# Exchanging real and imaginary state rows with a VectorE stream shuffle, two units at a time

## The chip, the cores and the metric

The kernel runs on one NeuronCore of a Trainium2 chip. The metric is the device time of one execution in microseconds (us). TensorE is called PE, VectorE DVE, ScalarE ACT, GpSimd POOL, and SP issues most of the DMAs.

## What is computed

Three layers follow one another: a gated linear attention with a complex decaying state, a mixture of experts that sends each token to one of 8 experts, and a bilinear layer. The change touches the first:

```python
# B=2, H=8, S=768, D=48; a is scaled to |a| <= 0.999
for t in range(S):
    new_re = ar * S_re - ai * S_im
    new_im = ar * S_im + ai * S_re
    S_re, S_im = new_re + outer(k[t], v[t]), new_im
    y[t] = q[t] @ S_re
x = moe(y)            # x @ w_gate, argmax, two matmuls per expert
out = (x @ w_a) * (x @ w_b) @ w_out
```

## The kernel before

The sequence is cut into 8 chunks of 96 steps, so there are 128 rows of (batch, head, chunk). A first stage on DVE (with ACT and PE helping) scans the decay factors inside all chunks at once (`scan`, L365) and multiplies keys and queries by them (`product`, L415 to L437). A product writes 12 time steps of 96 channels: for each step first 48 real numbers, then 48 imaginary ones. There are 16 products of 1152 elements per partition, one of them cut in three. The products are turned on PE so that the 96 channels lie on the partitions (`turn`, L454), and those of the keys also go to HBM (`x_rows`) and come back per chunk (`load_x`, L716).

The second stage, which this document calls the state stage, goes through 32 units of four heads; two successive units (n even, n + 1) share a chunk and a batch and are called a pair here, pairs 0 to 15. Pairs 0 to 7 belong to batch 0, pairs 8 to 15 to batch 1; the first pair of a batch (0 and 8) has no incoming state, the last (7 and 15) makes no outgoing one. The loop is at L876 to L928. What a unit does:

- `scores` (L696): 4 matmuls, keys times queries inside the chunk, issued one unit ahead; `masked` (L706): DVE masks them into SBUF.
- `state_in` (L821): 4 matmuls, keys times values; DVE adds the old state (L839, or copies where there is none, L841) into `zm[0]`, 96 partitions x 224.
- The state is multiplied by the chunk's complex decay. The real factor: DVE `zm[1] = zm[0] * Wr` (L910). The imaginary factor needs real and imaginary rows exchanged, with a sign: PE multiplies `zm[0]` by the constant matrix `swap` (`turned_state`, L869 to L874), DVE multiplies the result by `Wi` (L925), and DVE adds both into `Z[gr]` (L928), the state for the next chunk.
- `queried` (L844): 4 matmuls of masked scores with values, and for each, where a state came in, one of queries with the state (L857). ACT copies the outcome to SBUF (L865, L866).

Once a pair is finished, the tokens of its chunk are routed: DVE picks the expert (`choose`, L725), PE counts ranks (`ranks`, L746), DVE makes the slots (`place_chunk`, L756), and a POOL indirect DMA scatters the rows to `sorted_x` (L781). Routing of chunk 13 is followed by a load of expert 0's first rows from `sorted_x` (L919 to L921), which `turn_first` (L785) waits for at the end of the stage. Chunks 14 and 15 are added by `add_late`. Then the experts and the bilinear layer run, mostly on PE.

The order on each engine is the program order written out by hand in the loop; every engine works its queue in order and waits on semaphores. The decay factors of whole chunks, `Wr` and `Wi`, come from `end_factors` (L656), six DVE operations on `eT`, which ACT copied from PSUM (L607).

Of the kernel before, what the change touches and what calls it, by code (L numbers as in the profile page):

```python
# [24 lines left out]
ALU = mybir.AluOpType  # L25
# [43 lines left out]
def build(nc, dims, qk, v, vt, a, w_gate, w1, w2, wa, wb, wo, out, CAP):  # L69
    B, H, S, D = dims  # L70
    P = 128
# [31 lines left out]
    with ctx:  # L103
# [3 lines left out]
        def sb(name, shape, dt=F32, at=ctx, side="left"):  # L107
# [15 lines left out]
        swap = sb("swap", [C2, C2])  # L123
# [15 lines left out]
        m = pool.done(g.memset(swap[:], 0.0))  # L139
        pool.wait(m)  # L140
# [27 lines left out]
        with att:  # L168
# [86 lines left out]
            dve.done(vv.tensor_copy(trib[:], tri[:]))  # L255
            m_const = [dve.done(vv.tensor_scalar(baseb[:], basef[0:L], ident[0:L, 0:1], None, ALU.mult))]
# [158 lines left out]
            def product(s, x, n, cuts=1):  # L415
# [8 lines left out]
                for u in range(cuts):  # L424
# [3 lines left out]
                    m = dve.done(tt(walk(o, [D, 2], [2 * D if n else -2 * D, w], [1, D]),  # L428
# [165 lines left out]
            dve.done(vv.tensor_copy(ends[:, 2:4, :].rearrange("p i (r d) -> p i r d", r=2),  # L594
                                    walk(AT_Z[1] + lo_at + D, [SA, 2], [0, 2], [1, D])))
            dve.wait(m)
            dve.done(tt(ends[:, 0, :].rearrange("p (r d) -> p r d", r=2), both(tmp[:, 0, :]), both(tmp[:, 2, :]), ALU.add))
            m_ends = dve.done(tt(ends[:, 1, :].rearrange("p (r d) -> p r d", r=2), both(tmp[:, 3, :]),
# [8 lines left out]
            m_eT = act.done(ss.activation(eT[0:C2], bank[b][0:C2, :].rearrange("p (i q) -> p i q", i=4), ACT.Copy))  # L607
# [16 lines left out]
            AT_ST = AT_ZM + 3 * YB * DE  # L624
            AT_XS = AT_ST + NU * YB * DE
# [3 lines left out]
            zm = [flat(AT_ZM + i * YB * DE, YB * DE, C2) for i in range(3)]  # L629
            ws = [flat(AT_ENDS + i * P, P, C2) for i in range(2)]  # L630
            Z = [flat(AT_ST + i * YB * DE, YB * DE, C2) for i in range(NU)]
# [45 lines left out]
            z_done = [None] * NU  # L677
            rk = bank[0][:, 0:E]
            m_lgp, m_lx = {}, []

# [755 lines left out]
```

## Time and profile before

| | us |
|---|---|
| median of 3 runs | 593.72 (592.88 to 594.88) |
| profiled execution, time | 594.27 |
| profiled execution, span | 593.0 |
| PE busy | 548.9 (93%) |
| DVE busy | 375.5 (63%) |
| ACT busy | 266.0 (45%) |
| POOL busy | 51.8 (9%) |

The granted PE clock is 0.972 of full speed over the span. Up to about 118 us the first stage runs, from 120.5 to 218 us the state stage, then experts and the bilinear layer. Busy time is an average over stages with different limits, so the state stage has to be read by itself.

### The profile page before, as it was taken

To read this page: it belongs to the slowest core of one execution; us is meant where nothing else is said; L and a number is where in the kernel's file an instruction comes from. 1 tells how busy PE (TensorE), PEld (TensorE's weight loads), DVE (VectorE), ACT (ScalarE), POOL (GpSimd) and SP (SyncE) were. 2 spreads that over 40 slices of the span, in tenths; PEclk is the share of its full clock that TensorE was granted. 3 is DMA by queue.
4 is the path that set the end of the run, shared out by engine and by line. 5 is a ranking of instruction groups with operands and counts; after the bars stand their busy time and mean duration, and the time that the engine had idled before them with its cause. 6 is when DMAs were issued, how large, how long until landed. Compare 5 with 4: busy or idle time off the path is not lost.

```text
span 593.0 us, 10227 instructions
## 1 busy us (share of the span) xinstructions
PE 548.9 (93%) x3800; PEld 488.6 (82%) x3801; DVE 375.5 (63%) x938; ACT 266.0 (45%) x566; POOL 51.8 (9%) x66
## 2 busy tenths in 40 slices
PE   0499697889999999999999999999999999999996
PEld 0267364779999998999999998888888888888886
DVE  5999999968888869888889886534412212122121
ACT  5665665822222237777778784433232122322112
POOL 1000000001121116000000000350020000200002
PEclk9977897999999989999999999999999999999999
DMA  8999032497222125966666629730010000100001
GB/s 312 274 384 338 1 156 67 177 265 216 71 68 65 42 72 159 324 237 207 200 229 214 204 90 162 138 103 0 1 55 0 1 0 1 54 1 0 1 0 54
DMA packets 46321, 73.28 MB, mean 124 GB/s; under 512 B 16520, under 2 KB 38792, under 8 KB 45384
## 3 DMA queue, kind: packets, MB, share of 16 engines
q1 hardware_dynamic: 44360, 67.97, 37.0%
q0 software_dynamic: 1920, 4.75, 2.5%
q8 instruction: 28, 0.46, 0.3%
q14 instruction: 13, 0.11, 0.1%
HBM read 55.76 MB, written 16.97 MB: 123 GB/s over the span
## 4 chain that ended last, share of the span: by engine, by line
PE 79%; DVE 11%; ACT 4%; DMA 3%; issue 2%; POOL 1%; DVEq 0%; POOLq 0%; SPq 0%; ACTq 0%
PE psum L1330 26%; PE psum L1303 12%; PE psum L1136 11%; PE psum L1099 9%; PE psum L855 4%; PE psum L702 3%; PE psum L829 3%; PE psum L283 2%; PE psum L857 2%; PE psum L284 2%; DVE region L375 2%; PE psum L874 2%; DMA xrow<-sorted_x 2%; DVE region L428 2%; DVE region L380 1%
## 5 line engine op out<-in xcount | busy, mean ns | idle before, releaser
L1345 DVE TENSOR_TENSOR ga<-ga,psum 128x512 f32<-128x512 f32 x36 | 24.8, 688 | 129.8 <-PE psum L1330 124.7
L1349 ACT ACTIVATE gh<-ga 128x512 fp32r<-128x512 f32 x36 | 22.8, 632 | 80.7 <-DVE ga L1345 73.9
L1343 ACT ACTIVATE ga<-psum 128x512 f32<-128x512 f32 x36 | 21.5, 598 | 76.0 <-PE psum L1330 74.6
L283 PE MATMUL psum<-region,ident 128*128 128x384 f32 (+1 forms) x42 | 25.2, 692 | 32.7 <-ACT region L293 22.9
L1136 PE MATMUL psum<-hh,w2h 128*128 128x224 f32 x192 | 53.7, 279 | 0.0
L1099 PE MATMUL psum<-xh,w1h 128*128 128x224 f32 x192 | 53.0, 276 | 0.5 <-DVE xl L970 0.5
L1136 PE MATMUL psum<-hh,w2l 128*128 128x224 f32 x192 | 52.7, 274 | 0.0
L1099 PE MATMUL psum<-xh,w1l 128*128 128x224 f32 x192 | 52.7, 274 | 0.0
L1099 PE MATMUL psum<-xl,w1h 128*128 128x224 f32 x192 | 52.7, 274 | 0.0
L1136 PE MATMUL psum<-hl,w2h 128*128 128x224 f32 x192 | 52.6, 274 | 0.0
L1303 PE MATMUL psum<-woh,gh 128*128 128x384 f32 x144 | 48.3, 335 | 0.4 <-DVE gl L1351 0.4
L1303 PE MATMUL psum<-wol,gh 128*128 128x384 f32 x144 | 48.2, 335 | 0.0
L1303 PE MATMUL psum<-woh,gl 128*128 128x384 f32 x144 | 48.1, 334 | 0.0
L283 PEld LDWEIGHTS psum<-region,ident 128*128 128x128 f32 x42 | 10.6, 270 | 41.1 <-issue 21.3
L1330 PE MATMUL psum<-yh,wah 128*128 128x512 f32 x108 | 42.9, 397 | 0.0
L1330 PE MATMUL psum<-yh,wbh 128*128 128x512 f32 x108 | 42.8, 396 | 0.0
L1330 PE MATMUL psum<-yl,wah 128*128 128x512 f32 x108 | 42.8, 396 | 0.0
L1330 PE MATMUL psum<-yh,wal 128*128 128x512 f32 x108 | 42.6, 395 | 0.0
L1330 PE MATMUL psum<-yl,wbh 128*128 128x512 f32 x108 | 42.6, 395 | 0.0
L1330 PE MATMUL psum<-yh,wbl 128*128 128x512 f32 x108 | 42.6, 395 | 0.0
L1351 DVE TENSOR_TENSOR gl<-ga,gh 128x512 fp32r<-128x512 f32 x36 | 24.9, 693 | 25.2 <-ACT gh L1349 24.5
L1099 PEld LDWEIGHTS psum<-xh,w1h 128*128 128x128 f32 x192 | 36.9, 192 | 0.8 <-DVE xl L970 0.7
(198 smaller groups left out, 1461.4 us busy)
## 6 DMA issues: line engine op xcount, KB each, us to landing
raw<-w SPq DMA_DIRECT2D x14, 1536.0 KB, 6.7
sorted_x<-region SPq DMA_DIRECT2D x8, 579.0 KB, 13.7
queries<-qk SPq DMA_DIRECT2D x4, 1152.0 KB, 25.7
xrow<-sorted_x SPq DMA_DIRECT2D x7, 579.0 KB, 6.8
region<-x_rows SPq DMA_DIRECT2D x14, 288.0 KB
queries<-w SPq DMA_DIRECT2D x2, 1536.0 KB, 15.1
x_rows<-region SPq DMA_DIRECT2D x5, 576.0 KB, 2.8
region<-a SPq DMA_DIRECT2D x2, 1152.0 KB, 9.9
```

What stands on the lines that cost most here:

```text
L283: nc.tensor.matmul(x, ident[:], x0[:, cut], start=True, stop=False)
L702: m = nc.tensor.matmul(bank[2 + r][0:L, i * L:(i + 1) * L], XT[:, p, :], QT[:, p, :], start=True, stop=True)
L829: m = nc.tensor.matmul(bank[6][0:C2, i * DE:i * DE + 2 * D], XS[x_at % NXS][:, n % XB * YB + i, :], with_gate(p), start=True, stop=True)
L855: m = nc.tensor.matmul(o, SC[r][:, i, :], with_gate(p), start=True, stop=j == 0)
L1099: m = nc.tensor.matmul(bank[b][:, 0:cols], wx[:, c, f * P:(f + 1) * P], xx[:, c, 0:cols], start=c == 0 and i == 0, stop=c == KC - 1 and i ...
L1136: m = nc.tensor.matmul(bank[YB0 + c][:, 0:cols], wx[:, f, c * P:(c + 1) * P], xx[:, f, 0:cols], start=f == 0 and i == 0, stop=f == NF - 1 ...
L1303: m = nc.tensor.matmul(ot[s][:, 0:DM], gx[f % GB3][:, s * P:(s + 1) * P], wx[:, f, :], start=f == 0 and i == 0, stop=f == NF2 - 1 and i == 2)
L1330: m = nc.tensor.matmul(b_[:, 0:TT], wx[:, f, c, :], xx[:, c, t * TT:(t + 1) * TT], start=c == 0 and i == 0, stop=c == KC - 1 and i == 2)
L1343: m = act.done(ss.activation(ga[f % 2][:], ba[:, 0:TT], ACT.Copy))
L1345: m = dve.done(tt(ga[f % 2][:], ga[f % 2][:], bb[:, 0:TT], ALU.mult))
L1349: m = act.done(ss.activation(gh[f % GB3][:], ga[f % 2][:], ACT.Copy))
L1351: m_g.append(dve.done(tt(gl[f % GB3][:], ga[f % 2][:], z32(gh[f % GB3][:]), ALU.subtract)))
```

## The change

The sixteen products write real and imaginary parts interleaved (channel 2d real, 2d + 1 imaginary), as do the factors in `ends`. Real and imaginary partners are then neighbouring partitions, and DVE's stream shuffle with the lane list `i ^ 1` exchanges them; the matrix `swap`, its building on POOL, and the matmul are gone. The sign is put into the imaginary decay factor: `eT` is copied in two ACT operations, one with the per-partition scale `sign`. Two units are handled at once: the add, the shuffle, the imaginary product and the last add have 448 elements instead of 224, and the real product is done by ACT, in eight operations of 56 elements, each with a per-partition scale. `end_factors` moves in front of the first `masked`, the waits for the values behind the first two `scores`. In the loop, both `state_in` of a pair come first, the state's last add (`state_out`) moves into the second unit, and the ranks and slots of chunk 13 move ahead of `queried`.

```diff
-        swap = sb("swap", [C2, C2])
+        sign = sb("sign", [C2, C2])
...
-        m = pool.done(g.memset(swap[:], 0.0))
-        pool.wait(m)
+        pool.wait(m_ones)
...
-        c = pool.done(g.affine_select(out=swap[:], in_=swap[:], compare_op=ALU.not_equal, fill=1.0, base=-D,
-                                      pattern=[[-1, C2]], channel_multiplier=1))
-        pool.wait(c)
-        c_swap = pool.done(g.affine_select(out=swap[:], in_=swap[:], compare_op=ALU.not_equal, fill=-1.0, base=D,
-                                           pattern=[[-1, C2]], channel_multiplier=1))
...
+            SHUFFLE = [i ^ 1 for i in range(32)]
+            m = dve.done(vv.tensor_reduce(out=sign[:, 1:2], in_=ident[0:C2, 1:C2:2], axis=AXX, op=ALU.add))
+            dve.wait(m)
+            m_sign = dve.done(vv.tensor_scalar(sign[:, 0:1], sign[:, 1:2], -2.0, 1.0, ALU.mult, ALU.add))
...
-                    m = dve.done(tt(walk(o, [D, 2], [2 * D if n else -2 * D, w], [1, D]),
+                    m = dve.done(tt(walk(o, [1, 2], [2 * D if n else -2 * D, w], [2, D]),
                                     walk(AT_Z[1] + s * W + n * D + i0 * PAIR, [SA, 2], [PAIR, w], [1, D]),
                                     walk(k_at + i0 * PAIR, [0, 2], [PAIR, w], [1, D]), ALU.mult))
...
-            m_eT = act.done(ss.activation(eT[0:C2], bank[b][0:C2, :].rearrange("p (i q) -> p i q", i=4), ACT.Copy))
+            act.wait(m_sign)
+            by_i = bank[b][0:C2, :].rearrange("p (i q) -> p i q", i=4)
+            act.done(ss.activation(eT[0:C2, 0:4:2, :], by_i[:, 0:4:2, :], ACT.Copy))
+            m_eT = act.done(ss.activation(eT[0:C2, 1:4:2, :], by_i[:, 1:4:2, :], ACT.Copy, scale=sign[:, 0:1]))
...
-            nc.tensor.wait_ge(s_v[0], 16)
-            nc.tensor.wait_ge(s_vwin[0], 16)
-            pe.wait(c_swap)
+            m_factors = end_factors()
...
+            def added(n):
+
+                dve.wait(m_u[n + 1])
+                if units[n][0]:
+                    dve.wait(z_done[n - GB], m_zr[n - GB])
+                    m_add[n] = dve.done(tt(z_sum, Z[(units[n][0] - 1) % 2], state, ALU.add))
+                else:
+                    if m_zr:
+                        dve.wait(m_zr[max(m_zr)])
+                    m_add[n] = dve.done(vv.tensor_copy(z_sum, state))
+                act.wait(m_add[n], m_factors)
+                if z_done:
+                    act.wait(z_done[max(z_done)])
+                for r in range(GB):
+                    for i, p in enumerate(heads(n + r)):
+                        m_zr[n] = act.done(ss.activation(z_re[:, r, i, :], z_sum[:, r, i, :], ACT.Copy,
+                                                         scale=Wr[:, p:p + 1]))
+
+            def turned(n):
+
+                j, gr = units[n]
+                dve.wait(m_add[n])
+                m = dve.done(vv.stream_shuffle(z_im, z_sum, SHUFFLE))
+                dve.wait(m)
+                w = Wi[:, gr * YB * NC + j:(gr + GB) * YB * NC:NC].rearrange("c (r i) -> c r i", r=GB)
+                m_zi[n] = dve.done(tt(z_im, z_im, w.unsqueeze(3).broadcast_to([C2, GB, YB, DE]), ALU.mult))
+
+            def state_out(n):
+
+                dve.wait(m_zi[n], m_zr[n])
+                z_done[n] = dve.done(tt(Z[units[n][0] % 2], z_re, z_im, ALU.add))
...
-            def turned_state(n):
-
-                pe.wait(m_add[n])
-                if m_turned_z:
-                    pe.wait(m_turned_z)
-                return pe.done(nc.tensor.matmul(bank[7][0:C2, 0:YB * DE], swap[:], zm[0], start=True, stop=True))
...
+                if n == 0:
+                    nc.tensor.wait_ge(s_v[0], 16)
+                    nc.tensor.wait_ge(s_vwin[0], 16)
+                if more and n % GB == 0:
+                    for i in range(GB):
+                        state_in(n + i)
+                    added(n)
+                if n + 1 < NUNIT:
+                    masked(n + 1)
+                if n % GB == 0 and done == LATE - 1:
                     ranks(done)
                     place_chunk(done)
+                    first_rows()
+                if more and n % GB == 0:
+                    turned(n)
+                if n % GB and n > GB and done < LATE - 1:
+                    place_chunk(done)
+                if more and n % GB:
+                    state_out(n - 1)
+                queried(n)
+                if n % GB == 0 and n and done != LATE - 1:
                     ranks(done)
-                if more:
-                    m_j = turned_state(n)
-                    dve.wait(m_j)
-                    m_turned_z = m_jd[n] = dve.done(tt(z3[2], bank[7][0:C2, 0:YB * DE].rearrange("p (i e) -> p i e", i=YB),
-                                                       wv(Wi), ALU.mult))
-                    dve.wait(m_jd[n], m_zr, m_y[n])
-                    z_done[gr] = dve.done(tt(z3[3], z3[1], z3[2], ALU.add))
+                    if done >= LATE:
+                        place_chunk(done)
```

## Rows read from the trace of the kernel before

**Rows 1.** The page's chain that ended last, shares of the span.

```profile
PE 79%; DVE 11%; ACT 4%; DMA 3%; issue 2%; POOL 1%; DVEq 0%; POOLq 0%; SPq 0%; ACTq 0%
```

**Rows 2.** Busy us (xinstructions) by window: pairs 1-6, 8, 9, 10-13; clock, DMA, GB/s.

```profile
127.91:166.07 38.16, 38.16 (x426) 37.54 (x425) 32.34 (x121) 7.76 (x36) 4.79 (x5) 1.00 0.54 158
...
170.29:175.37 5.08, 5.08 (x58) 4.98 (x57) 3.92 (x17) 1.51 (x8) 1.39 (x2) 1.00 0.11 32
175.37:181.96 6.59, 6.58 (x72) 6.34 (x71) 5.82 (x22) 1.36 (x8) 0.93 (x1) 1.00 0.34 87
181.96:207.44 25.48, 25.48 (x286) 25.06 (x284) 21.48 (x81) 5.31 (x25) 3.68 (x4) 1.00 0.20 55
```

**Rows 3.** PE in order of time, inside pair 4: start, duration, operation.

```profile
146.55 0.58 PE L874 MATMUL psum<-region,swap 96*96 96x224 f32 x2
146.97 0.84 PE L702 MATMUL psum<-region 96*96 96x96 f32 x8
...
148.32 0.33 PE L855 MATMUL psum<-region 96*96 96x96 f32 x2
...
149.65 0.58 PE L874 MATMUL psum<-region,swap 96*96 96x224 f32 x2
```

**Rows 4.** DVE in order of time, same pair; brackets: idle before, releaser.

```profile
147.90 0.26 DVE L729 TENSOR_REDUCE route<-region 96x8 f32<-96x64 f32 x1
...
148.97 0.38 DVE L839 TENSOR_TENSOR region<-region,psum 96x224 f32<-96x224 f32 x1
...
151.62 0.38 DVE L839 TENSOR_TENSOR region<-region,psum 96x224 f32<-96x224 f32 x1 [0.55 <-PE psum L829]
151.93 0.15 DVE L760 TENSOR_TENSOR so<-so,ohb 96x8 bf16<-96x8 bf16 x1
...
152.52 0.38 DVE L910 TENSOR_TENSOR region<-region 96x224 f32<-96x224 f32 x1
```

**Rows 5.** DVE in order of time at the state stage's start.

```profile
119.39 0.69 DVE L473 COPY region<-psum 96x512 f32<-96x512 f32 x1 [1.59 <-PE psum L465]
...
124.08 0.57 DVE L712 COPY_PREDICATED region<-mask,psum 96x384 f32<-96x384 int32 x1
124.55 0.27 DVE L658 TENSOR_TENSOR region<-region 96x127 f32<-96x127 f32 x1
```

**Rows 6.** DVE groups by form: xcount, busy us, mean ns of one, idle before.

```profile
L428 DVE TENSOR_TENSOR region<-region,queries 128x1152 f32<-128x1152 f32 x10 | 13.1, 1352 | 0.1
...
L928 DVE TENSOR_TENSOR region<-region 96x224 f32<-96x224 f32 x28 | 10.9, 388 | 1.0
...
L729 DVE TENSOR_REDUCE route<-region 96x8 f32<-96x64 f32 x16 | 4.1, 258 | 1.6 <-ACT region L865 1.6
...
L1272 DVE TENSOR_REDUCE gate<-past 128x12 f32<-128x96 f32 x1 | 0.3, 253 | 0.0
...
L1355 DVE TENSOR_SCALAR gate<-tag 128x12 f32<-128x12 f32 x1 | 0.2, 167 | 0.0
```

**Rows 7.** ACT groups by form, the same columns.

```profile
L1179 ACT ACTIVATE yh<-psum 128x384 f32 x24 | 10.3, 492 | 18.3 <-PE psum L1099 13.7 <-PE psum L1136 4.6
...
L1375 ACT ACTIVATE raw<-psum,gate 128x384 f32<-128x384 f32 x12 | 6.6, 582 | 6.5 <-PE psum L1303 6.5
...
L865 ACT ACTIVATE region<-psum 96x32 f32<-96x32 f32 x32 | 6.2, 193 | 54.7 <-PE psum L857 45.5 <-PE psum L855 9.2
```

**Rows 8.** PE in order of time at the stage's start and at pair 1.

```profile
120.51 1.57 PE L702 MATMUL psum<-region 96*96 96x96 f32 x16 [1.16 <-DMA region<-vw_rows]
...
127.91 0.84 PE L702 MATMUL psum<-region 96*96 96x96 f32 x8
```

**Rows 9.** The chain of waits at the stage's end: start, us, what.

```profile
212.09 2.56 DMA sorted_x<-region,sloti
...
214.72 3.84 DMA region<-sorted_x
```

**Rows 10.** PE in order of time, the first operation after those loads.

```profile
218.60 2.93 PE L791 MATMUL psum<-ident,region 128*128 128x128 f32 x12 [0.62 <-DMA region<-sorted_x]
```

More of the change, by code:

```diff
@@ L628, in build @@
             maski = mask[:].bitcast(I32).unsqueeze(1).broadcast_to([L, YB, L])
-            zm = [flat(AT_ZM + i * YB * DE, YB * DE, C2) for i in range(3)]
+            z_sum, z_re, z_im = (flat(AT_ZM + i * PW, PW, C2).rearrange("p (r i e) -> p r i e", i=YB, e=DE) for i in range(3))
             ws = [flat(AT_ENDS + i * P, P, C2) for i in range(2)]
-            Z = [flat(AT_ST + i * YB * DE, YB * DE, C2) for i in range(NU)]
+            Z = [flat(AT_ST + i * PW, PW, C2).rearrange("p (r i e) -> p r i e", i=YB, e=DE) for i in range(2)]
+            state = psum[0:C2, 6:8, 0:YB * DE].rearrange("p r (i e) -> p r i e", i=YB)
             X = flat(AT_Z[1], TAU * ROW, L).rearrange("p (t c) -> p t c", c=ROW)
@@ L671, in build @@
             assert GB == XB and B == 2
-            m_scored, m_sc, m_u, m_y, m_yx, m_add, m_jd = ({} for _ in range(7))
+            m_scored, m_sc, m_u, m_y, m_yx, m_zr, m_zi, m_add = ({} for _ in range(8))
             m_oh, m_slot, m_rk, m_tk, m_so, m_hot, m_part_x, m_read_lg = ({} for _ in range(8))
@@ L828, in state_in @@
                 for i, p in enumerate(heads(n)):
-                    m = nc.tensor.matmul(bank[6][0:C2, i * DE:i * DE + 2 * D],
-                                         XS[x_at % NXS][:, n % XB * YB + i, :], with_gate(p),
-                                         start=True, stop=True)
+                    m = nc.tensor.matmul(bank[6 + r][0:C2, i * DE:i * DE + 2 * D], XS[x_at % NXS][:, r * YB + i, :],
+                                         with_gate(p), start=True, stop=True)
                 m_u[n] = pe.done(m)
-                if n % XB == XB - 1 and x_at + NXS < NX:
+                if r == GB - 1 and x_at + NXS < NX:
@@ L851, in queried @@
                 if j:
-                    pe.wait(z_done[gr])
+                    pe.wait(z_done[n - r - GB])
                 for i, p in enumerate(heads(n)):
@@ L893, in build @@
                         sp.dma_start(y.rearrange("p (c f) -> p c f", f=x.shape[-1]), x).then_inc(s_, 16)
-                if more and n:
-                    state_in(n)
-                if n % GB == 1 and n > GB and done < LATE - 1:
+                if n == 0:
[5 more added lines that the diff above has]
+                    added(n)
@@ L897, in build @@
+                if n + 1 < NUNIT:
+                    masked(n + 1)
+                if n % GB == 0 and done == LATE - 1:
                     ranks(done)
                     place_chunk(done)
-                if n == 0:
-                    queried(0)
-                    state_in(0)
-                    masked(1)
-                    m_ends = end_factors()
-                z3 = [x.rearrange("p (i e) -> p i e", i=YB) for x in (*zm, Z[gr])]
-                def wv(x):
-                    return x[:, gr * YB * NC + j:(gr + 1) * YB * NC:NC].unsqueeze(2).broadcast_to([C2, YB, DE])
@@ L908, in build @@
-                if more:
-                    dve.wait(m_add[n], m_ends)
-                    m_zr = dve.done(tt(z3[1], z3[0], wv(Wr), ALU.mult))
-                if n:
-                    if n + 1 < NUNIT:
-                        masked(n + 1)
-                    queried(n)
-                if n % GB == 0 and done >= LATE - 1:
-                    ranks(done)
-                    place_chunk(done)
-                    if done == LATE - 1:
-                        sp.wait_ge(pe.sem, m_y[NUNIT // 2 - 1][1])
-                        sp.wait_ge(s_sc, 16 * LATE)
-                        sp.dma_start(rows_0, sorted_x[0, 0:CAP, :].rearrange("(i p) c -> p i c", p=P)).then_inc(s_row0, 16)
@@ L990, in build @@
             pe_done, dve_done = (pe, pe_chunks, False), (dve, dve_chunks, False)
-            act.wait(m_y[NUNIT - 1], *z_done)
-            dve.wait(*z_done)
+            act.wait(m_y[NUNIT - 1], *z_done.values())
+            dve.wait(*z_done.values())
             nc.scalar.wait_ge(s_w1, 16)
```

33 lines of the change are left out of this document (15 added, 18 removed).

## The prediction

> **What bounds the kernel now.** I read the shares of the chain that ended last first, then the state stage by windows, then single engines in order of time inside one pair. PE holds 79% of the chain and DVE 11% [rows 1]. In the state stage PE is busy in all of 38.16 us of pairs 1 to 6 and all of 25.48 us of pairs 10 to 13, at full granted clock, so a pair costs 6.36 to 6.37 us [rows 2]. DVE is busy 32.34 of 38.16 us (85%), and in each pair it idles 0.55 us for a PE result [rows 4]: it is behind PE, but not far. What the exchange costs on PE is the step from one `swap` matmul to the next work, 146.55 to 146.97, 0.42 us, twice in a pair [rows 3]. A group of four 96x96 matmuls costs 0.68 us (two groups in 146.97 to 148.32), a `queried` with incoming state 1.33 us (148.32 to 149.65) [rows 3]. Pairs 0, 8 and 9 are not steady: 7.40 us from the first `scores` to pair 1 [rows 8], 5.08 and 6.59 us [rows 2].
>
> **PE's side of the change.** Two swaps go: 0.84 us in a pair, which leaves 6.37 - 0.84 = 5.53 us. Pairs 1 to 6 give 5.04 us and pairs 10 to 13 give 3.36. Pair 7 has no outgoing state: nothing. Pair 8 holds six groups of four (0.68 each) and the ranks (what is left of 6.37 after 0.84, 4 x 0.68 and 2 x 1.33, about 0.15): 4.2 us instead of 5.08, gain 0.88. Pair 9 should take the steady 5.53 instead of 6.59, gain 1.06. In pair 0 PE now has seven groups in a row, 4.76 us: no state comes in, `end_factors` is no longer between an add and its product, and the second `queried` doesn't wait for a chain of DVE work; gain 2.64 from 7.40. The first `scores` waited for `vw_rows` (1.16 us idle) [rows 8]. Now they wait only for the last copy of the first stage, which ends at 119.39 + 0.69 = 120.08 [rows 5]; PE starts near 120.2 instead of 120.51, gain 0.3. Sum: 0.3 + 2.64 + 5.04 + 0.88 + 1.06 + 3.36 = 13.3 us.
>
> **Whether DVE keeps up.** An operation of 224 elements takes 388 ns, one of 1152 takes 1352 [rows 6], so 1.04 ns per element, and one of 448 takes 0.62 us; 0.08 less to the next one that waits for nothing (0.38 us long, the next after 0.31) [rows 4]. The trace has no shuffle. At twice the element rate it would be about 0.4 us, as several passes over 32 partitions 1.9; I take 0.62, the row of the same size, since it too reads and writes each element once. A pair then costs DVE: `choose` 1.07 (147.90 to 148.97) and `place_chunk` 0.59 (151.93 to 152.52) [rows 4], two masks at 0.47 (124.08 to 124.55) [rows 5], add 0.54, shuffle with its wait 0.65, product 0.54, last add 0.54: 4.87 us, 0.66 below PE.
>
> The Trainium skill ("VectorE: DVE Perf Modes", the perf-mode tier table) gives the shuffle one element per cycle, about 2400 ns for 2048 elements; my estimate from that page is 0.73 us for 448. No row here shows it, and the sum would stay as it is.
>
> **The order of waits in a pair.** Time 0 is the pair's first `scores` on PE. PE: scores 0.68, both `state_in` to 2.04, `queried` to 3.37, ranks and scores to 4.20, `queried` to 5.53. DVE starts the add when `state_in` is done, 2.25, then mask, shuffle, product to 4.45, mask, slots, last add from 5.5 to 6.13 (0.60 of the next pair), `choose` to 7.15, and would be ready 0.6 before the next add. The new state is needed by PE at 2.04 of the next pair, 1.4 us later. Behind `state_out` on DVE are `choose` and the next add; behind them PE waits for nothing before its next `state_in`.
>
> ACT's eight small operations are on no row. 32 elements take 193 ns, 384 take 492, and a per-partition scale adds 90 (582) [rows 7]: about 0.30 each, 2.4 us if none overlaps, about 1.2 with the closest overlap. They run from 2.9 to between 4.1 and 5.3; `state_out` asks at 5.5. Hidden at both ends, cover 0.2 to 1.4 us. The two result copies of `queried` queue behind them and are needed only two units later.
>
> **Edits taken at nothing.** Pair 14: the end is set by another chain. The scatter of chunk 13 (2.56 us) and the load of the first rows (3.84 us) follow one another, and PE idles 0.62 us for them [rows 9, 10]. The slots of chunk 13 still come about 3.9 us into pair 14 (before behind `queried`, now behind the 448-element add and a mask), so that chain moves with the start of the pair; PE's swaps saved in pair 14 only lengthen its idle time to about 1.4 us. The opening has fewer POOL operations and two more small DVE ones; the copy of `eT` is split in two. These, and a lower clock after the longer idle, could cost 0 to 1.5 us; I take 0.6.
>
> **The product's new write order.** Sixteen products of 1152 elements write every second word instead of runs of 48. DVE works without a gap there, so any price counts, less about 1 us in the third slot, which waits for ACT afterwards. No row writes so. For reads, rows of both kinds exist: L1355 reads every second word and takes 167 ns for 12 elements, just what 388 ns - 212 x 1.04 gives for contiguous ones; L729 reads every eighth word, and takes 258 ns for 64 elements where L1272 has 253 for 96 contiguous, so 38 ns too much, 0.6 ns per element [rows 6]. Ends: nothing; 0.6 ns, which is 16 x 1152 x 0.6 = 11.1, less 1, 10 us; or one more cycle, 1.04 ns, 18 us. I take nothing, for L1355 has the same step, though as a read and on few elements.
>
> The Trainium skill is of two minds. "SBUF — State Buffer" (Door 1) says two accesses within 16 bytes keep full rate; a step of two words does that, and L1355 agrees. "Vector Engine (DVE) Microarchitecture Reference" (5.2) wants runs of two adjacent words, on the written side too, and has 1.71 instead of 1.05 ns per element for a destination that hops each time: by that estimate 11 us of the 13 are given back, and L729's excess is of that size.
>
> **Forecast.** 13.3 less 0.6 is 12.7. The profiled execution at 594.27 lies 0.55 above the median of the runs, 593.72; from the median the forecast is 581.0, its own range 579 to 583.5.
>
> **Rivals.**
> 1. Strided writes cost about 0.6 ns per element (L729 speaks for it, L1355 against). 581.0 + 10 = 591; 588 to 594 with the size in doubt.
> 2. The other side: each strided write takes a further full cycle, 18 us, 599. It decides from (12.7 + 1) / 18432 = 0.74 ns per element; below that the kernel is not slower. For it: every element is then an access of its own. Against: no row shows that much.
> 3. The loop is bound by DVE or by ACT's small operations instead of PE. The shuffle has 0.66 us of slack, each us above costs 12 (the 12 pairs with both adds and routing); as three passes over 32 partitions, 1.9 us, it costs 0.6 x 12 = 7, 588. ACT decides only if its eight take over 3.2 us, 0.4 each (the next add has 0.6 to spare beyond the 5.5). Ahead of pair 4, loads of `x_rows` queued behind the expert's weights could also come late, since the pair comes 5 us sooner. 584 to 590, middle 586.
> 4. The shuffle costs over 2.3 us and the stage gets slower than before: over 595. Or the stage isn't bound by PE as read; then nothing changes. Both unlikely, 85% DVE and 100% PE being plain.
>
> **Chances.** Forecast 0.55; rival 1 0.22; rival 2 0.06; rival 3 0.12; rival 4 0.05 (half slower, half the same). About 0.3% (1.8 us) is what this kernel's measurement can tell from no change: 592 to 595.5. Of rival 1, 0.14 is faster, 0.05 the same, 0.03 slower. Faster: 0.55 + 0.12 + 0.14 = 0.81. Same: 0.05 + 0.02 = 0.07. Slower: 0.06 + 0.03 + 0.03 = 0.12. The range is 579 to 593.
>
> **What would show it.** Right: no PE matmul of the old L874; PE busy throughout pairs 1 to 6 with about 33.1 us for the six; DVE idle for `state_in` once a pair, some 0.6 us; the shuffle near 0.6 to 0.75 us; ACT's eight ending before `state_out`; L428's mean still near 1352 ns; pair 1 starting 4.8 us after the first `scores`; PE idle about 1.4 us before `turn_first`. Wrong: L428 at 2 us or more and the state stage starting 10 us later; PE idle before `queried` for a state, or pairs of 6 us with DVE busy throughout.

## The result, and the profile after

The changed kernel takes 587.79 us (median of its runs), the kernel before in the same comparison 594.3 us; the ratio is 0.9901, interval 0.9873 to 0.9928. The change is worth 6.5 us by the medians (5.9 by the ratio) where 12.7 were forecast. The profiled execution took 588.88 us with a span of 587.6; its span is 5.4 us shorter than that of before (593.0). It is the third of four: two others took 586.7 us. In some comparisons below single executions fell in a slower state (10 to 27 us longer at a lower granted clock); the ratios and intervals leave them out, the medians don't.

The state stage first, since the forecast was made there. The windows of the changed kernel, columns as in [rows 2] (window, its length, then PE, weight loads, DVE, ACT and POOL busy, clock, DMA, GB/s): pair 0, pairs 1 to 6, 7, 8, 9, 10 to 13, 14, and pair 15 up to `turn_first`; the last line is expert 1's first layer.

```profile
120.20:125.40 5.20, 5.03 (x56) 4.89 (x57) 3.49 (x12) 1.16 (x5) 0.00 (x0) 1.00 1.13 261
125.40:159.30 33.90, 33.65 (x404) 33.48 (x403) 29.69 (x104) 20.03 (x90) 4.77 (x5) 1.00 0.74 202
159.30:163.60 4.30, 4.30 (x54) 4.28 (x53) 3.09 (x14) 1.32 (x6) 0.92 (x1) 1.00 0.11 34
163.60:167.90 4.30, 4.30 (x54) 4.30 (x53) 3.14 (x11) 2.26 (x10) 1.39 (x2) 1.00 0.30 75
167.90:173.50 5.60, 5.60 (x70) 5.60 (x69) 5.36 (x19) 3.74 (x19) 0.92 (x1) 1.00 0.37 103
173.50:195.80 22.30, 22.30 (x271) 22.30 (x269) 19.75 (x73) 12.93 (x58) 3.67 (x4) 1.00 0.21 56
195.80:201.40 5.60, 5.60 (x70) 5.60 (x68) 4.85 (x18) 3.18 (x14) 1.73 (x2) 1.00 0.10 29
201.40:207.35 5.95, 3.84 (x48) 3.71 (x46) 4.28 (x21) 2.81 (x12) 0.43 (x1) 1.00 0.38 125
235.69:247.07 11.38, 11.38 (x74) 11.38 (x75) 7.09 (x14) 6.82 (x15) 0.00 (x0) 0.71 0.50 191
```

A pair costs 22.30 / 4 = 5.58 us instead of 6.37, with PE busy in all of it: PE still sets the pace, as in [rows 2], and the 0.8 us of the two swaps are gone. DVE in order of time inside one pair answers to [rows 4], and below it comes ACT with the eight small operations of the real factor:

```profile
150.42 0.62 DVE L838 TENSOR_TENSOR region<-region,psum 96x448 f32<-96x448 f32 x1 [0.51 <-PE psum L827]
150.96 0.58 DVE L711 COPY_PREDICATED region<-mask,psum 96x384 f32<-96x384 int32 x1
151.44 0.01 DVE L855 LOAD_MASK_SELECT region<-region  x1
151.44 0.66 DVE L855 STREAM_SHUFFLE region<-region 96x448 f32<-96x448 f32 x1
152.14 0.62 DVE L858 TENSOR_TENSOR region<-region 96x448 f32<-96x448 f32 x1
...
153.75 0.61 DVE L863 TENSOR_TENSOR region<-region 96x448 f32<-96x448 f32 x1
...
156.00 0.62 DVE L838 TENSOR_TENSOR region<-region,psum 96x448 f32<-96x448 f32 x1 [0.50 <-PE psum L827]
```

```profile
151.07 1.97 ACT L848 ACTIVATE region<-region 96x56 f32<-96x56 f32 x8 [1.10 <-DVE region L838]
```

The shuffle takes 0.66 us, ACT's eight operations 1.97 us, over at 153.04, 0.7 us before the last add (153.75) that reads them. DVE idles 0.50 us a pair for the incoming state. The products with the new write order, by form over the whole program, answer to L428 in [rows 6]:

```profile
L424 DVE TENSOR_TENSOR region<-region,queries 128x1152 f32<-128x1152 f32 x10 | 13.1, 1354 | 0.1
```

They take 1354 ns against 1352 ns before: writing every second word costs nothing.

Then the end of the stage, and what comes behind it. These are the idle times of PE from 118 to 250 us, by line: engine, line, what it waited for, total us, times, longest.

```profile
PE psum L1107 <- DVE yl L1189: 2.4, 1, 2.4
PE psum L790 <- DMA region<-sorted_x: 2.1, 1, 2.1
...
PE psum L827 <- DMA region<-x_rows: 0.4, 2, 0.3
```

PE in order of time, the first line of `turn_first` [rows 10] and of expert 1's first layer:

```profile
207.35 0.82 PE L790 MATMUL psum<-ident,region 128*128 128x128 f32 x5 [2.11 <-DMA region<-sorted_x]
...
235.69 0.55 PE L1107 MATMUL psum<-xh,w1h 128*128 128x224 f32 x1 [2.37 <-DVE yl L1189]
```

`turn_first` starts 218.60 - 207.35 = 11.25 us earlier than before. So the stage kept 11.25 us, and what comes behind it gave 5.85 back. I followed how far single matmuls of the changed kernel lie ahead of the same ones of the kernel before: 11.15 us when expert 0 starts, 10.75 from 229 us on (times of the changed kernel), 8.2 when expert 1's first layer starts (235.69 against 243.91), 5.04 when that layer is done (247.07 against 252.11), 5.4 at the end. The two large steps are at one place. Expert 1's first layer takes 11.38 us at a granted clock of 0.71 in the changed kernel; in the kernel before it takes 8.20 at full clock:

```profile
243.91:252.11 8.20, 8.20 (x76) 8.20 (x75) 7.27 (x16) 7.55 (x18) 0.00 (x0) 1.00 1.05 381
```

The clock records put 6.8 us at half clock (1.2 instead of 2.4 GHz) from 235.4 on, right behind the 2.37 us for which PE was idle.

The view blames that idle time on DVE's `yl`, which had just ended. But the kernel before starts the same layer at 243.91 us, 0.9 us ahead of the same `yl`, so the layer doesn't need it:

```profile
244.84 1.49 DVE L1181 TENSOR_TENSOR yl<-psum,yh 128x384 f32 x3 [1.79 <-ACT yh L1179]
```

The raw records of PE's sequencer, which the busy rows leave out, show another cause. `sized` writes every layer of an expert twice, for 384 columns and for 224, and jumps over one of them:

```python
with nc.tensor.If(n > PART):
    body(CAP)
with nc.tensor.Else():
    body(PART)
```

The records of this branch, start in us and duration in ns (a few of each kernel):

```
before  L1066   225.693  241    234.391  353    242.691   335    251.491  223
after   L1074   223.290  213    231.944 3499                     246.210  213
```

One of them takes 3499 ns, all the others of this line 0.2 to 0.4 us. It ends at 235.44, and the first matmul follows 0.25 us later (and again 0.25 us in the three kernels below in which it is slow too). PE's queue of matmuls lasts until 235.69 - 2.37 = 233.32, so it covers 1.4 us of the branch; the rest is idle. The instruction queue tells what differs. It brings packets of 16 KB, and PE works through some 256 instructions from one to the next: in the kernel before, from 444 us on, 254 to 257 matmuls, weight loads and sequencer records. In the kernel before one such packet comes at 236.7, six us ahead of the branch; in the changed kernel it comes at 232.9, while the branch is already waiting. The DMA queues show it in the stretch 231.9 to 235.7 of the changed kernel, and in 236 to 238 of before:

```profile
q8 instruction: 1, 0.02, 1.9%
```

```profile
q8 instruction: 1, 0.02, 3.0%
```

Up to this branch PE has 3418 records in the kernel before and 3304 in the changed kernel, 114 fewer: 28 swaps of two matmuls and two weight loads each, and two waits. So everything behind has moved against these blocks of 256. That is a theory about an address, and it can be tested.

### The profile page after: what moved, and what is told of

Read it like the earlier page. It is cut to its first block, busy times and chain, and to the rows that moved or that the text cites. A ratio compares the mean times of both kernels' runs of the same rounds, so it can differ in the third digit from the quotient of the medians.

```text
span 587.6 us, 10183 instructions
## 1 busy us (share of the span) xinstructions
PE 540.6 (92%) x3744; PEld 482.2 (82%) x3745; DVE 369.2 (63%) x898; ACT 292.1 (50%) x679; POOL 52.0 (9%) x63
## 4 chain that ended last, share of the span: by engine, by line
PE 76%; DVE 12%; DMA 6%; ACT 4%; issue 1%; POOL 0%; SPq 0%; DVEq 0%; ACTq 0%; POOLq 0%
PE psum L1338 26%; PE psum L1311 12%; PE psum L1144 10%; PE psum L1107 10%; PE psum L876 3%; DMA region<-x_rows 3%; PE psum L701 3%; PE psum L827 3%; DVE region L371 2%; PE psum L878 2%; PE psum L279 2%; DVE region L424 2%; DVE region L376 1%; PE psum L280 1%; DMA raw<-w 1%
## 5 line engine op out<-in xcount | busy, mean ns | idle before, releaser
L1107 PE MATMUL psum<-xh,w1h 128*128 128x224 f32 x192 | 54.6, 284 | 2.9 <-DVE yl L1189 2.4
L1107 PE MATMUL psum<-xl,w1h 128*128 128x224 f32 x192 | 54.1, 282 | 0.0
L1107 PE MATMUL psum<-xh,w1l 128*128 128x224 f32 x192 | 54.1, 282 | 0.0
L1107 PEld LDWEIGHTS psum<-xh,w1h 128*128 128x128 f32 x192 | 38.3, 199 | 3.4 <-DVE yl L1189 2.5
```

Source lines behind the costliest of these rows:

```text
L1107: m = nc.tensor.matmul(bank[b][:, 0:cols], wx[:, c, f * P:(f + 1) * P], xx[:, c, 0:cols], start=c == 0 and i == 0, stop=c == KC - 1 and i ...
```

## The experiments

**The position of the code.** Three kernels differ from the changed one (e1, e2) or the one before (e3) in nothing but small matmuls in the opening, before PE has other work. A matmul is two instructions, since it brings its weight load; 57 of them give back the 114.

```diff
+            pe.wait(m_ones)
+            for i in range(57):
+                nc.tensor.matmul(bank[7][0:8, 0:8], onesb[:, 0:8], onesb[:, 0:8], start=True, stop=True)
```

e1, the changed kernel with 57 (the position of before):

> The changed kernel with 57 tiny bf16 matmuls (114 instructions, a weight load and a matmul each) on PE in the opening, where PE has nothing to do; its PE program is then as long as that of the kernel before, so the branch in front of expert 1's first matmuls stands at the same place of the instruction stream as there. Theory (code position: the changed kernel's COMPARE_BRANCH at expert 1 took 3.50 us instead of 0.34 because its target's code was fetched only then): the branch takes 0.2 to 0.4 us, PE doesn't idle 2.4 us, the half-clock stretch of 6.8 us goes, 5.6 us gained: about 582.2 us against 587.8 for the changed kernel, ratio to before 0.980. Rival (the branch was slow because the weight loads had the DMA engines busy, or by chance): the slow branch stays, 588, ratio 0.990. Second rival (the loads' timing makes PE wait anyway): the branch is fast but a wait for weights takes its place, 586 or more.

e2, the changed kernel with 128, a whole block of 256 instructions further, as a control:

> The changed kernel with 128 tiny matmuls (256 instructions, one 16 KB code fetch's worth) in the opening: the control for the padding. By the theory of code position the place within a fetch is that of the changed kernel, so the branch at expert 1 again takes about 3.5 us and the time is 587 to 588, ratio 0.990. If the padding itself helped (a warmer clock, another start), or only the order of events in time mattered, it would be as fast as the kernel padded by 114, about 582.

e3, the kernel before with 71, which makes 142 = 256 - 114 instructions and so the position of the changed kernel:

> The kernel before with 71 tiny matmuls (142 instructions; 142 + 114 = 256) in the opening, so that its branch at expert 1 stands within a 16 KB fetch where the changed kernel's does. Theory of code position: its branch takes about 3.5 us, PE idles and runs at half clock afterwards, 5.6 us lost: about 599.5 us, ratio 1.009. Rival (something else of the changed kernel delays the branch): no difference, 594, ratio 1.000.

Measured: e1 586.71 us, ratio 0.9895 (0.9860 to 0.9931); e2 587.35, ratio 0.989 (0.9871 to 0.9909); e3 598.36, ratio 1.0074 (1.0058 to 1.0089). The branch ahead of expert 1's first layer in each, start and duration as above:

```
e1   235.081  335        e2   231.198 3534        e3   242.854 3554
```

and PE's idle times from there on show in e3 the wait that the kernel before doesn't have:

```profile
PE psum L1103 <- DVE yl L1185: 2.4, 1, 2.4
```

So the position of the code decides whether the branch is slow. Counted from the kernel before, -114 and +142 are slow and 0 is fast, as a period of 256 instructions has it. The packets say why: in the four profiles with a slow branch (changed, e2, e3, e9 below) the instruction packet starts 0.9 to 1.1 us after the branch; in those with a fast one (before, e1, e5, e6, e8) the last packet came 6.0 to 6.9 us ahead of it. That the loads of the expert's weights fill the DMA queues at this time is not what makes the branch slow, since they fill them in the kernel before and in e1 too; whether they lengthen the 3.5 us was not tried. To price the slow branch I matched ACT's copies of the experts' results out of PSUM one by one with those of the kernel before. What each kernel has at 261 us it has at 502 us too, to 0.1 us; what each loses between 244 and 261 us is the branch with its clock (the shift is time minus time of before):

| kernel | shift at 244 us | at 261 us | lost | half clock behind the branch |
|---|---|---|---|---|
| changed | -10.75 | -5.41 | 5.3 | 6.8 us |
| e2 | -11.50 | -7.58 | 3.9 | 3.4 us |
| e3 | +0.16 | +2.47 | 2.3 | none |
| e1 | -7.61 | -7.62 | 0.0 | none |

The wait itself is worth 2.3 us, and the clock behind it 0, 1.6 or 3.0 at the same code position. The profiled execution of e3 was the fastest of its six; the median of all is 598.36 - 593.59 = 4.8 us above before. Where the others lost the rest is open: their mean granted clocks (0.968 to 0.973) are about that of the profiled one (0.969), so more half clock doesn't explain all of them.

But e1, with a short branch, is not measurably faster than e2 or the changed kernel: the ratios are 0.9895, 0.989 and 0.9901, and the 582.2 us written down for it were missed by 4.5. Its profile shows where the gain went: its shift was only 7.6 us before the experts began. At the start of the state stage PE waited for the first load of `x_rows`:

```profile
122.08 1.18 PE L831 MATMUL psum<-region 96*96 96x96 f32 x6 [0.87 <-DMA region<-x_rows]
```

and from there it stood at half clock for 6.8 us (122.1 to 129.0). The window of pair 0 and part of pair 1:

```profile
119.60:129.57 9.97, 9.06 (x66) 8.96 (x67) 5.63 (x17) 2.67 (x12) 0.00 (x0) 0.66 1.04 239
```

Pair 1's first `state_in` came at 129.40 instead of 126.10. In the changed kernel the first `state_in` waited 0.17 us for that load and the clock stayed; the kernel before came there at 122.9 and never waited for it. Nor did e3, and yet it stood at half clock for the same 6.8 us (122.1 to 129.0):

```profile
120.00:130.00 10.00, 9.46 (x65) 8.67 (x66) 5.25 (x16) 0.82 (x4) 0.00 (x0) 0.66 0.96 229
```

**The first load.** e6 is e1 with pair 0 in another order: the second mask and `queried(0)`, which need no `x_rows`, come ahead of the first `state_in`, and `end_factors` behind that mask.

```diff
-            m_factors = end_factors()
...
                 if n == 0:
                     nc.tensor.wait_ge(s_v[0], 16)
                     nc.tensor.wait_ge(s_vwin[0], 16)
+                    masked(1)
+                    queried(0)
+                    m_factors = end_factors()
                 if more and n % GB == 0:
                     for i in range(GB):
                         state_in(n + i)
                     added(n)
-                if n + 1 < NUNIT:
+                if n and n + 1 < NUNIT:
                     masked(n + 1)
...
-                queried(n)
+                if n:
+                    queried(n)
```

> The changed kernel with the 57 small matmuls of e1, and pair 0 reordered: the mask of unit 1 and queried(0) come before the first state_in, and end_factors only after that mask. TensorE then has about 0.7 us more work between its first scores and the first operand that the load of x_rows brings. My theory: the 0.87 us wait for that load in e1 (state_in at 122.08) and the half clock right behind it (122.1 to 128.9) are one thing, cost e1 3 to 4 us, and vanish here: state_in without a wait for the load, full clock in pair 1, pair 1's first state_in near 126 instead of 129.4, span 581 to 583, median 582 to 584, some 11 us below the kernel before. Rival A: the half clock comes anyway (it is bound to another moment than the wait), then the median stays at 586 to 588 with a half-clock stretch somewhere in 115 to 135 us. Rival B: the stage gains its 4 us, but the loads of the experts and the chain at the stage's end don't come earlier and take it back: pair 9 earlier by 3 to 4 us, the end by less than 1.5 us.

Measured: 585.06 us, ratio 0.9852 (0.9831 to 0.9874), span of the profiled execution 582.6. PE in order of time:

```profile
121.90 0.89 PE L880 MATMUL psum<-region 96*96 96x96 f32 x8
122.63 1.52 PE L831 MATMUL psum<-region 96*96 96x96 f32 x16
```

There is no wait for the load, no half clock between 115 and 208 us, and 2.8 us less span than in e1; the time is 0.6 us (by the ratio) to 1 us (by the median) above what I had written. The other executions fit: the mean granted clock is 0.968 to 0.972 in five of e6's six, and 0.958 to 0.967 in all of e1's. That the wait and the half clock are one thing is not shown: e5 below waited 0.8 us for the same load and kept its clock, and e3 fell without that wait. e9 is then the same without the 57 matmuls (the branch stands ahead of expert 1's first layer, not its second, as the text on record has it):

> e6 without the 57 small matmuls, so that TensorE's program is 114 instructions shorter again, as in the changed kernel. My theory: the two losses are separate. The branch ahead of expert 1's second layer takes 3.5 us again instead of 0.3, TensorE idles 2.4 us and then has 3.4 to 6.8 us of half clock; pair 0 and 1 stay at full clock. Median 586.5 to 588.5, 3 to 4 us over e6. The rival: the 3 us between e6 and e1 came from something else in the reordering, and the branch costs nothing that the next load doesn't hide: then 584 to 585.5.

Measured: 587.93 us, ratio 0.988 (0.9843 to 0.9916), span 587.8. The branch took 3679 ns at 233.39, and PE in order of time has the wait behind it:

```profile
237.32 0.36 PE L1111 MATMUL psum<-xh,w1h 128*128 128x224 f32 x1 [2.55 <-DVE yl L1193]
```

From 244 to 261 us it lost 4.1 us (its shift goes from -9.30 to -5.24), with 3.4 us of half clock; e6 lost nothing there (-10.47, -10.45). So in the profiles the two losses are separate. With neither cured the ratio is 0.9901, with the code's position alone 0.9895, with the order alone 0.988, with both 0.9852. The intervals of the first three overlap; both together are 0.5% better than the changed kernel, and there the intervals only touch. The two profiled spans (582.6 against 587.6 us) overstate it, since one is of e6's fastest execution and the other of the third of four. e9 and e6 overlap as well: two of e9's six executions took 584.3 and 584.5 us at a mean clock of 0.975, the others up to 591.3 at 0.961. What the branch costs is read from the profiles, and from e3 as a whole; the ratios of e1 and e9 alone don't show it.

**The end of the stage.** In the changed kernel PE idles 2.1 us for the load of expert 0's rows (2.7 in e6), and the clock is at half for 3.4 us from there. In e8 the ranks and slots of chunk 13 are placed between pair 14's two `state_in`, ahead of the add:

```diff
-                    for i in range(GB):
-                        state_in(n + i)
+                    state_in(n)
+                    if done == LATE - 1:
+                        ranks(done)
+                        place_chunk(done)
+                        first_rows()
+                    state_in(n + 1)
                     added(n)
...
-                if n % GB == 0 and done == LATE - 1:
-                    ranks(done)
-                    place_chunk(done)
-                    first_rows()
```

> e6 with the ranks and slots of chunk 13 (and the load of the first expert's rows behind them) placed ahead of the last add of the state, between its two state_in, instead of behind it and a mask. In e6 the slots were ready at 199.91 us, TensorE idles 2.7 us before turn_first and then runs at half clock for 3.4 us. My theory: the chain from choose(13) over the scatter and the load of the first rows sets the start of the experts; the slots come 1.2 to 1.5 us sooner, TensorE waits 0.3 us for the ranks in pair 14 but that much less at turn_first, and the end comes 1.0 to 1.8 us sooner (median 582.8 to 583.8 where e6 had 584.6 in its undisturbed runs). The rival: the rest of the chain (the scatter after its own queue's work, the loads of the second expert's weights) is not moved by it; then the end stays within 0.5 us of e6.

Measured: 582.59 us, ratio 0.9776 (0.9749 to 0.9802), 12 us (by the medians) to 13 us (by the ratio) below the kernel before. The interval is clear of e6's (0.9831 to 0.9874), so this gain holds beyond the profiles. `turn_first` in e6, then in e8, PE in order of time:

```profile
208.02 0.46 PE L793 MATMUL psum<-ident,region 128*128 128x128 f32 x1 [2.66 <-DMA region<-sorted_x]
```

```profile
209.64 1.61 PE L793 MATMUL psum<-ident,region 128*128 128x128 f32 x12
```

From the start of pair 14 to the start of `turn_first` it is 208.02 - 195.97 = 12.05 us in e6 and 209.64 - 199.80 = 9.84 in e8. The load of the rows starts 7.70 us into pair 14 in e6 and 6.10 in e8, and takes 4.31 and 3.69 us. There is no gap long enough for the view to name a releaser, and the clock stays whole: the twelve matmuls take 1.61 us instead of 2.81 in e6. To the first matmul of expert 0 it is 19.68 us in e6 and 15.92 in e8, a gain of 3.8 us: 2.2 from the wait and the rest from the clock. I had put the gain at 1.0 to 1.8: the wait was undersized, and the clock left out. The two profiled executions have the same span only because that of e8 lost 2.9 us in the opening (its first `scores` is at 123.11 instead of 120.18, with 34 us at half clock ahead of 105 us instead of 27) and waited 1.0 for `x_rows` in pair 4.

**The shuffle without the pairing.** e4 is the kernel before with interleaved rows and a shuffle for each unit; 43 small matmuls keep the code's position (3417 records ahead of the branch). It was run a second time, as e4b, for its profile.

```diff
-                    m_j = turned_state(n)
-                    dve.wait(m_j)
-                    m_turned_z = m_jd[n] = dve.done(tt(z3[2], bank[7][0:C2, 0:YB * DE].rearrange("p (i e) -> p i e", i=YB),
-                                                       wv(Wi), ALU.mult))
+                    m = dve.done(vv.stream_shuffle(zm[2], zm[0], SHUFFLE))
+                    dve.wait(m)
+                    m_jd[n] = dve.done(tt(z3[2], z3[2], wv(Wi), ALU.mult))
```

> The kernel before with only the exchange replaced: interleaved layout, sign in the factors and a stream shuffle of 224 elements per unit instead of the swap matmul; loop order, real product on DVE and units one by one as before; 43 tiny matmuls in the opening keep PE's program as long as before, and with it the branch. My theory of the state stage: DVE had 5.5 us of work in a pair of 6.37; two shuffles of about 0.43 with their waits make it 6.3 to 6.4, so DVE takes PE's place as the bound and next to nothing is gained: 592 to 596, ratio 0.997 to 1.003. Rival (PE's work alone decides): 0.84 us less in twelve pairs, 584, ratio 0.983. The product's write order is here too: L424's form should stay at 1352 ns.

> The kernel of e4 again, for a profile of an undisturbed execution: interleaved rows and a stream shuffle for each unit (224 elements) in the kernel before, no pairing of the units' state. Span near 593 to 596 us. If the exchange on TensorE (0.42 us twice a pair) was the whole gain, a pair should fall to 5.5 to 5.6 us here too; if the chain of a single unit (state_in, add, product, shuffle, last add, queried) now has to fit between two TensorE groups, TensorE idles before queried for the state and a pair costs 6 us or more.

Measured: 595.97 us, ratio 1.0035 (1.0019 to 1.005): 0.35% slower than before. The profile is of e4b (597.11 us, span 595.9). Its pairs 10 to 13 take 25.16 us, 6.29 each, and this is the window with PE's waits in it (DVE has none there):

```profile
183.65:208.81 25.16, 23.80 (x272) 23.07 (x270) 23.62 (x98) 4.85 (x24) 3.68 (x4) 1.00 0.22 59
```

```profile
PE psum L832 <- DVE region L842: 1.4, 4, 0.3
```

DVE is now busy in 23.62 of 25.16 us (94%; before 84%), since it has twice as many operations as the paired version, each with its fixed part, and PE waits for its add once in each pair. The swaps' 0.84 us shrink to 6.37 - 6.29 = 0.08. So the gain needs both: the shuffle takes PE's swaps away, and the pairing keeps DVE below PE. In this execution `turn_first` starts 2.75 us later than before: 1.07 are there at the first `scores` (2.4 us of waiting for `vw_rows`), 0.63 come in pair 0, which stands at half clock, pairs 1 to 13 give 0.33 back, and pairs 14 and 15 lose 1.38.

**The real factor on DVE.** e5 is e1 with one product of 448 elements on DVE instead of ACT's eight operations.

```diff
-                act.wait(m_add[n], m_factors)
...
-                        m_zr[n] = act.done(ss.activation(z_re[:, r, i, :], z_sum[:, r, i, :], ACT.Copy,
-                                                         scale=Wr[:, p:p + 1]))
...
+                m_zr[n] = dve.done(tt(z_re, z_sum, wr.unsqueeze(3).broadcast_to([C2, GB, YB, DE]), ALU.mult))
```

> e1 with the real-factor product as one VectorE operation of 448 elements between the shuffle and its product, instead of ScalarE's eight small ones. VectorE then has about 4.9 + 0.6 = 5.5 us of work in a pair of 5.58 us that TensorE needs. My theory: TensorE still sets the pair; the stage grows by 0 to 1.5 us in all 12 pairs, median 586.5 to 588.5. The rival (VectorE and the chain add, shuffle, products, last add bind the pair as soon as 0.6 us is put on VectorE): 0.3 us or more in each of 12 pairs, 4 us or more in all, over 590, with TensorE idle for the state in each pair.

Measured: 586.86 us, ratio 0.9885 (0.9866 to 0.9903), not to be told from e1. The window of four of its pairs:

```profile
178.85:201.20 22.35, 22.35 (x270) 22.21 (x268) 21.16 (x76) 5.31 (x24) 3.67 (x4) 1.00 0.21 59
```

PE is busy throughout, 5.59 us a pair, with DVE at 95%; ACT's share of the work left DVE 0.35 us a pair more room (19.75 against 21.16 us busy in four). In such pairs, moving the real factor to ACT brought nothing. Elsewhere in the stage the two profiles differ: from pair 1 to `turn_first` e5 takes 83.91 us and e1 82.41. Pairs 7 and 9 take 0.4 us more each in e5, pair 4 takes 0.2 and pairs 14 and 15 together 0.7, while e1 loses 0.2 in pair 1, which begins at half clock. The two executions are alike only because pair 0 takes 5.94 us in e5 and 8.85 in e1, at half clock. So the real factor on ACT may be worth some 1.5 us, the upper end of what I had written; one profile of each doesn't prove it.

**What a step costs.** e7 has a chain of DVE operations on scratch data, all 96 x 448: destination step 1, 2, 4, 8 on L263, 265, 267, 269, source step 2, 4, 8 on L271, 273, 275, the kernel's own order on L277. Its time (611.51 us) holds the chain and is not compared.

> e1 with a chain of VectorE operations on scratch data at the start of the opening, each of 96 partitions x 448 fp32 elements unless said: products with a destination step of 1, 2, 4 and 8 words, products with a source step of 2, 4 and 8 words, the kernel's own order (halves interleaved word by word), a stream shuffle of 448, a copy of 448, a stream shuffle of 224 and of 64 elements. The theory that a step of two words is free and a longer one is not: steps 1 and 2 within 10 ns of each other (about 0.61 us), steps 4 and 8 longer, 0.6 ns per element or so (0.88 us). The rival (no step costs anything; the 38 ns of the routing line before had another cause): all alike. Shuffle 448 at 0.66 us as in the changed kernel, 224 at 0.40, and 64 gives the fixed part: about 0.22 us if it is the same as that of a product, or up to 0.3.

The groups by form, columns as in [rows 6]:

```profile
L269 DVE TENSOR_TENSOR region<-region 96x448 f32<-96x448 f32 x2 | 1.9, 962 | 0.1
L275 DVE TENSOR_TENSOR region<-region 96x448 f32<-96x448 f32 x2 | 1.9, 954 | 0.1
L267 DVE TENSOR_TENSOR region<-region 96x448 f32<-96x448 f32 x2 | 1.9, 946 | 0.1
L273 DVE TENSOR_TENSOR region<-region 96x448 f32<-96x448 f32 x2 | 1.9, 942 | 0.1
...
L279 DVE STREAM_SHUFFLE region<-region 96x448 f32<-96x448 f32 x2 | 1.3, 641 | 0.0
L265 DVE TENSOR_TENSOR region<-region 96x448 f32<-96x448 f32 x2 | 1.2, 622 | 0.1
L271 DVE TENSOR_TENSOR region<-region 96x448 f32<-96x448 f32 x2 | 1.2, 622 | 0.1
L277 DVE TENSOR_TENSOR region<-region 96x448 f32<-96x448 f32 x2 | 1.2, 622 | 0.1
L263 DVE TENSOR_TENSOR region<-region 96x448 f32<-96x448 f32 x2 | 1.2, 621 | 0.1
...
L283 DVE STREAM_SHUFFLE region<-region 96x224 f32<-96x224 f32 x2 | 0.8, 395 | 0.0
...
L285 DVE STREAM_SHUFFLE region<-region 96x64 f32<-96x64 f32 x2 | 0.4, 218 | 0.0
```

Step 2 is free on either side; step 4 adds 325 ns, 0.73 ns per element where I had written 0.6, and step 8 hardly more. A shuffle takes about 147 ns and 1.10 ns per element (from 218 and 641 ns). The Trainium skill, "SBUF — State Buffer" (Door 1), has full rate for two accesses to the same 16-byte line; the trace agrees, for reads and for writes (622 ns at step 2, 946 and 942 at step 4). The Trainium skill, "Vector Engine (DVE) Microarchitecture Reference" (5.2), wants runs of two adjacent words; for steps of two words the same 622 ns don't bear that out.

## Why the prediction was right about the stage and wrong about the time

The terms, forecast against measured, up to `turn_first`:

| term | forecast us | measured us |
|---|---|---|
| first `scores` earlier | 0.3 | 120.51 - 120.15 = 0.36 |
| pair 0 | 2.64 | 7.40 - 5.27 = 2.13 |
| pairs 1 to 6 | 5.04 | 38.16 - 33.89 = 4.27 |
| pair 7 | 0 | 4.22 - 4.32 = -0.10 |
| pair 8 | 0.88 | 5.08 - 4.28 = 0.80 |
| pair 9 | 1.06 | 6.59 - 5.62 = 0.97 |
| pairs 10 to 13 | 3.36 | 25.48 - 22.32 = 3.16 |
| pairs 14, 15 | 0 | 11.16 - 11.50 = -0.34 |
| sum | 13.3 | 11.25 |

- That PE sets the stage, and the price of a swap: right. A pair is 5.58 us, 0.05 above the forecast. Pair 4 took 6.07 us, 0.5 more, since its `state_in` waited for `x_rows` (a load that took 15.5 us, 127.66 to 143.17, issued behind the expert's weights); rival 3 had named this. In e8 pair 4 took 6.82.
- DVE keeps up: right. Shuffle 0.62 taken, 0.66 measured; DVE idle for `state_in` 0.50 us a pair, 0.6 said. e4 shows how little was to spare, e5 that a further product of 448 elements in each pair was free in pairs 10 to 13, and that the whole stage from pair 1 on took 1.5 us more with it.
- ACT's eight operations hidden: right, 1.97 us in the bounds of 1.2 to 2.4.
- The strided write at nothing: right (1354 ns against 1352, and e7). Rivals 1 and 2 fell. L729's 38 ns, which spoke for rival 1, fit its step of eight words (in e7 a source step of eight adds 0.74 ns per element, 48 ns for L729's 64); L1355, which has the change's step of two, was the row to follow.
- Pair 14 hidden by the chain of the scatter and the load: right in kind. PE's idle time grew from 0.62 to 2.11 us, to 1.4 by forecast; the load of the rows started 7.75 us into pair 14, before 7.28, where no delay was forecast. e8 shows that this chain was mine to price: it could be shortened, for 3.8 us.
- The stage's sum was 2.05 us too large (13.3 against 11.25), most of it in pairs 1 to 6 (0.77), pair 0 (0.51) and pairs 14 and 15 (0.34).
- The step that failed is in "Edits taken at nothing": beyond the end of the stage, all that is left of the program was taken to move as a block, with 0.6 us of allowance for the opening and for "a lower clock after the longer idle". In the profiled execution it gave back 5.85 us, of which 2.55 lie at a branch that waited for its instructions and 3.16 in the half clock behind it (0.5 go ahead of it, 0.4 of that while the load of expert 1's weights stands in the chain for 7.71 us; 0.36 are regained). The clock that the allowance was for cost nothing: 3.4 us of half clock follow the longer idle time, and the same 3.4 us stand there in the kernel before. No rival held the branch. It is a cost of how many instructions stand ahead, not of the work: e3 has it with the kernel before, e1 and e6 are free of it with the changed one. That curing it alone (e1) didn't make the kernel faster shows that this loss doesn't stand alone: e1 lost some 3 us at the stage's start instead, to a wait for `x_rows` and half clock behind it.

The time is inside the range of 579 to 593, but the range was built from rivals that didn't happen; rival 3's 586 is close to it by chance.

Left open: what decides whether half clock follows a wait, and for how long. Behind the branch it was 6.8, 3.4, 3.4 us and none (changed, e2, e9, e3). At the stage's start e1, e3 and e4b had 6.8 us of it, e7 3.4 and the others none, and the small matmuls in the opening don't tell them apart (all four have them, but e2, e5, e6 and e8 too). Whether the opening's half clock (27 to 34 us) depends on anything in the program was not tried either. It moves single executions by some us, so one profile of each kernel can't be subtracted from another without looking at these stretches first.

## What to carry to other kernels

An edit that removes instructions also moves all code behind it. Where the time of a change falls short, look at the sequencer's own records for one branch or jump that takes microseconds while its twins take 0.3, compare the instruction queue's packets, and undo the move with as many cheap instructions as were removed, before doubting the model of the stage. Behind a PE wait of one to three microseconds some executions here lost up to 3 us more to half clock; in e8, removing the 2.7 us of idle time ahead of the experts brought 3.8. And an exchange taken from the bounding engine to its neighbour pays only if the neighbour has the room: the same shuffle saved 0.8 us a pair when two units shared each operation, and 0.1 when they didn't.

## What the runs showed of the hardware

- A branch whose instruction packet started only 0.9 to 1.1 us after it took 3.50, 3.53, 3.55 and 3.68 us in four kernels, against 0.2 to 0.4 us elsewhere. The instruction queue brings 16 KB a packet, one for each 254 to 257 instructions of PE. Shifting the changed kernel by 256 instructions leaves the branch slow, by 114 makes it fast; shifting the kernel before by 142 makes it slow.
- The clock after a wait is not settled by its length: half clock for 6.8 us behind 0.87 us of waiting in e1, none behind 0.8 in e5 and 1.0 in e8, and 6.8, 3.4 or none behind the same 2.4 us at the branch. In e3 it fell for 6.8 us from 122.1 on, behind a wait of 1.2 us for `vw_rows` that the kernel before has too, at full clock.
- A stream shuffle across neighbouring partitions costs little more than a product of its size (0.64 to 0.66 us against 0.62 for 96 x 448), and the load of its mask 14 ns at most.
- A step of two fp32 words is free for VectorE in reads and writes (622 ns against 621 for 96 x 448); a step of four costs 0.73 ns per element more (946 ns).
